# Pooled attention and two gated layers on one core: the first layer in blocks of 512 tokens instead of 288

## What is computed

```python
k_p = k.reshape(B, H, Sp, pool, D).mean(axis=3)
v_p = v.reshape(B, H, Sp, pool, D).mean(axis=3)
scores = scale * np.matmul(q, k_p.transpose(0, 1, 3, 2))
...
x = attn_out.transpose(0, 2, 1, 3).reshape(B * S, H * D)     # 4608 tokens x 512
h = x @ w_in                                                 # 512 -> 2048
g = np.where(h >= 1, h, np.where(h <= -1, 0.0, (h + 1) ** 2 / 4))
x = g @ w_out                                                # 2048 -> 512
h = x @ w_in2; g = h - np.tanh(h); y = g @ w_out2
```

## Time and profile before

| | us |
|---|---|
| median of 3 runs (1745.31 to 1745.89) | 1745.83 |
| the profiled execution | 1748.94 |
| its span, first to last instruction | 1747.0 |
| PE busy in it | 1709.3 (98%) |
| PE weight load busy | 1570.2 (90%) |
| DVE busy | 876.1 (50%) |
| ACT busy | 545.9 (31%) |
| POOL busy | 167.7 (10%) |
| mean granted TensorE clock | 0.993 of 2.4 GHz |
| chain that ended last, PE's share | 95% |

### The profile page before, as it was taken

The page is one execution under the profiler, slowest core; times in us unless marked ns, Lnnn a source line. Parts: engine busy times, 40 slices in busy tenths (PEclk is TensorE's granted clock), DMA queues, the critical chain, the costliest instruction groups (busy, mean ns, idle before and its releaser), DMA issues.

```text
span 1747.0 us, 24514 instructions
## 1 busy us (share of the span) xinstructions
PE 1709.3 (98%) x10480; PEld 1570.2 (90%) x10480; DVE 876.1 (50%) x1745; ACT 545.9 (31%) x1141; POOL 167.7 (10%) x136
## 2 busy tenths in 40 slices
PE   4999999999999999999999999999999999999998
PEld 4999999999999999999999888888888888888887
DVE  6585776767757768677554232323232323232322
ACT  3533333333333333333335222222222222222221
POOL 4610110011100110111007100000000000000000
PEclk7999999999999999999999999999999999999999
DMA  4512012002111020201024101010100000000000
GB/s 162 162 51 79 24 31 77 29 25 69 40 65 40 14 80 27 79 20 36 15 86 141 43 10 39 13 36 15 34 17 32 19 30 21 28 23 27 24 1 24
DMA packets 47628, 78.12 MB, mean 45 GB/s; under 512 B 3488, under 2 KB 19872, under 8 KB 47520
## 3 DMA queue, kind: packets, MB, share of 16 engines
q1 hardware_dynamic: 47520, 76.56, 13.5%
HBM read 57.67 MB, written 18.87 MB: 44 GB/s over the span
## 4 chain that ended last, share of the span: by engine, by line
PE 95%; DVE 3%; ACT 1%; POOL 0%; DMA 0%; issue 0%; DVEq 0%; SPq 0%
PE acc_ps L499 44%; PE h_ps L490 32%; PE att_ps L490 7%; PE score_ps L490 6%; PE score_ps L514 3%; PE score_ps L534 1%; PE att_ps L526 1%; DVE k_diag L850 1%; PE att_ps L534 0%; PE score_ps L535 0%; DVE g_lo L812 0%; DVE bent L819 0%; ACT bent L675 0%; DVE v_sum L861 0%; POOL win_lo L446 0%; DMA stage<-kT 0%
## 5 line engine op out<-in xcount | busy, mean ns | idle before, releaser
L499 PE MATMUL acc_ps<-g_hi,wout_hi 128*128 128x288 f32 (+1 forms) x1600 | 536.1, 335 | 2.1 <-DVE g_lo L812 2.1
L499 PE MATMUL acc_ps<-g_hi,wout_lo 128*128 128x288 f32 (+1 forms) x1600 | 526.0, 329 | 0.0
L499 PE MATMUL acc_ps<-g_lo,wout_hi 128*128 128x288 f32 (+1 forms) x1600 | 525.9, 329 | 0.0
L490 PE MATMUL h_ps<-x_hi,win_hi 128*128 128x288 f32 (+1 forms) x1248 | 400.9, 321 | 7.8 <-POOL win_lo L446 3.6
L490 PE MATMUL h_ps<-x_hi,win_lo 128*128 128x288 f32 (+1 forms) x1248 | 395.2, 317 | 0.0
L490 PE MATMUL h_ps<-x_lo,win_hi 128*128 128x288 f32 (+1 forms) x1248 | 395.1, 317 | 0.0
L499 PEld LDWEIGHTS acc_ps<-g_hi,wout_hi 128*128 128x128 f32 x1600 | 301.1, 188 | 25.4 <-DVE g_lo L812 2.4
L499 PEld LDWEIGHTS acc_ps<-g_lo,wout_hi 128*128 128x128 f32 x1600 | 301.1, 188 | 22.5
L499 PEld LDWEIGHTS acc_ps<-g_hi,wout_lo 128*128 128x128 f32 x1600 | 300.7, 188 | 22.3
L490 PEld LDWEIGHTS h_ps<-x_hi,win_hi 128*128 128x128 f32 x1248 | 234.9, 188 | 21.2 <-DVE g_lo L812 4.6
L490 PEld LDWEIGHTS h_ps<-x_lo,win_hi 128*128 128x128 f32 x1248 | 235.1, 188 | 11.2
(11 more groups left out here) (125 smaller groups left out, 1828.1 us busy)
## 6 DMA issues: line engine op xcount, KB each, us to landing
stage<-kT SPq DMA_DIRECT2D x16, 576.0 KB, 5.1
q_sb<-qT SPq DMA_DIRECT2D x16, 576.0 KB, 3.9
x2T_scratch<-prob SPq DMA_DIRECT2D x16, 576.0 KB, 3.4
x_lo<-x2T_scratch SPq DMA_DIRECT2D x9, 1024.0 KB, 7.3
yT<-out_sb SPq DMA_DIRECT2D x9, 1024.0 KB, 5.1
stage<-v SPq DMA_DIRECT2D x8, 1024.0 KB, 8.3
stage<-w_in SPq DMA_DIRECT2D x8, 1024.0 KB, 5.1
stage<-w_out SPq DMA_DIRECT2D x8, 1024.0 KB, 5.4
```

What stands on the lines that cost most here:

```text
L490: last = nc.tensor.matmul(h_bank(j, layer)[:, 0:WIDTH[layer]], w[:, c, j * P:(j + 1) * P], x[:, c, 0:WIDTH[layer]], start=(c == 0 and i == ...
L499: last = nc.tensor.matmul(acc_ps[:, m, 0:WIDTH[layer]], w[:, j, m * P:(m + 1) * P], g[:, j % GRING, 0:WIDTH[layer]], start=(j == 0 and i = ...
```

## The change

**Layer 1 in 9 blocks of 512 tokens.** T is 512 in both layers. Batches have 576 tokens, so a block no longer lies in one batch: block n holds the last 64 n tokens' worth of batch n - 1 and the first 512 - 64 n of batch n. `chunks(n)` cuts it into chunks of up to 128 queries of one batch: 4 where the border falls on a multiple of 128, else 5 (two of them of 64 queries); that is 5 for n = 1, 3, 5, 7 and 4 for the rest, 40 in all. `regions(n)` gives the one or two column ranges of a mix. Pooled K and V have two buffers, of the two batches.

**Attention.** Score units of a block use two PSUM banks in turn (`score_bank`), two units to a step from step 2. Turns and mixes stand at steps 9 to 14, the last three mixes and the last turn at steps 13 and 14. DVE makes `pool_k` in steps 0 and 1. POOL makes all of V's sums, by halving, tail included (`halve_v`), and DVE's `sum_v` is gone.

**x held once.** `x_hi` and `x_lo` have one buffer. `round_x1` of the next block waits until the last first product of this block is done.

**Weights where they land.** A piece of weights is loaded over the place of its low copy (`win_raw` and `win_lo` are the same memory); ACT casts it into the high copy and POOL subtracts in place. At the start SP issues all 8 pieces right behind K, Q and V, without a wait. In the last block of layer 1 a piece is loaded as soon as the piece that it replaces was last used. `q_sb` shares memory with the turned probabilities, so the next queries are loaded when the mixes are done.

```diff
-T = SEQ // 2
-BLOCKS = BATCH * SEQ // T
 TOKENS = BATCH * SEQ
-T2 = 512
-TP = 320
-LINE = 64
-BLOCKS2 = TOKENS // T2
-NEED2 = -(-T2 // T)
-CH = 96
-CHUNKS = T // CH
...
+T = 512
+BLOCKS = TOKENS // T
+SHIFT = SEQ - T
...
+def chunks(n):
+    edge = SHIFT * n
+    out = []
+    for c in range(T // P):
+        lo, hi = c * P, (c + 1) * P
+        if hi <= edge:
+            out.append((lo, P, n - 1))
+        elif lo >= edge:
+            out.append((lo, P, n))
+        else:
+            out.append((lo, edge - lo, n - 1))
+            out.append((edge, hi - edge, n))
+    return out
+def regions(n):
+    edge = SHIFT * n
+    return [r for r in [(0, edge, n - 1), (edge, T - edge, n)] if r[1] > 0]
...
-        x_hi = at("x_hi", X_AT, [P, 2, KT, TP], F32R)
-        x_lo = at("x_lo", X_AT + 2 * KT * TP, [P, 2, KT, TP], F32R)
...
+        win_raw = nc.alloc_sbuf_tensor_at("win_raw", [P, KT, FF], F32, offset=nc.lookup_mloc(win_lo.name).addr)
+        wout_raw = nc.alloc_sbuf_tensor_at("wout_raw", [P, FT, D], F32, offset=nc.lookup_mloc(wout_lo.name).addr)
+        x_hi = at("x_hi", X_AT, [P, KT, T], F32R)
+        x_lo = at("x_lo", X_AT + KT * T, [P, KT, T], F32R)
...
+        q_sb = at("q_sb", PT_AT, [P, PAIRS, T])
+        probT_hi = at("probT_hi", PT_AT, [P, PRING, T], F32R)
+        probT_lo = at("probT_lo", PT_AT + PRING * T, [P, PRING, T], F32R)
...
+        UNIT0_BANKS = [score_ps, h_ps[:, 0], h_ps[:, 1], acc_ps[:, 0], acc_ps[:, 1], acc_ps[:, 2], acc_ps[:, 3], att_ps]
+        def score_bank(n, k):
+            return UNIT0_BANKS[k] if n == 0 else [att_ps, score_ps][k % 2]
+        FIRST_STEPS = {0: 3, 1: 4, 2: 5, 3: 6, 4: 7}
+        SWITCH_STEPS = {2: 0, 5: 1, 6: 2, 9: 3, 10: 4, 13: 5, 14: 6}
...
             load_k(0)
-            load_q(0, 0)
+            load_q(0)
             load_v(0)
+            for i in range(NW):
+                load_w(1, i)
...
+            load_k(1)
+            sp.wait_ge(mixed, PAIRS)
+            load_q(1)
+            for blk in range(BLOCKS - 1):
+                n = blk + 1
+                if n < BATCH:
+                    sp.wait_ge(k_pooled, n + 1)
+                    load_v(n)
+                if n + 1 < BATCH:
+                    sp.wait_ge(v_split, n + 1)
+                    load_k(n + 1)
+                if n + 1 < BLOCKS:
+                    sp.wait_ge(mixed, PAIRS * (n + 1))
+                    load_q(n + 1)
                 store_out(blk)
...
+            def halve_v(b):
+                pool.wait_ge(v_loaded, 16 * (b + 1))
+                pool.wait_ge(v_tail_loaded, 16 * 2 * VTAIL_LOADS * (b + 1))
+                raw = v_raw(b).rearrange("p (i e) -> p i e", i=VTILES)
+                for level, width in enumerate([VE // 2, VE // 4, VE // 8]):
+                    if level > 0:
+                        pool.wait_ge(v_halved, 2 * b + level)
+                    if width > DH:
+                        nc.gpsimd.tensor_tensor(raw[:, :, 0:width], raw[:, :, 0:width], raw[:, :, width:2 * width],
+                                                ALU.add).then_inc(v_halved, 1)
+                    else:
+                        nc.gpsimd.tensor_tensor(v_sum[:], raw[:, :, 0:width], raw[:, :, width:2 * width],
...
-            for c in range(CHUNKS):
+            halve_v(0)
+            for c in range(len(chunks(0))):
                 normalise(0, c)
-            for i in range(4):
+            for i in range(6):
                 split_w(1, i)
-            normalise(1, 0)
-            split_w(1, 4)
-            normalise(1, 1)
-            split_w(1, 5)
-            normalise(1, 2)
-            split_w(1, 6)
-            split_w(1, 7)
-            for n in range(2, BLOCKS):
-                for c in range(CHUNKS):
+            for n in range(1, BLOCKS):
+                if n < BATCH:
+                    halve_v(n)
+                for c in range(len(chunks(n))):
                     normalise(n, c)
+                if n == 1:
+                    split_w(1, 6)
+                    split_w(1, 7)
...
+                    pe.wait_ge(k_pooled, min(n, BATCH - 1) + 1)
+                if n > 0 and k >= 2:
+                    pe.wait_ge(shift_done, GROUPS * before(n) + k - 1)
...
+                    last = nc.tensor.matmul(score_bank(n, k)[0:rows, e * 2 * KEYS:(e + 1) * 2 * KEYS],
+                                            q_sb[:, p, first:first + rows], k_diag[:, b % 2, p, :], start=True, stop=True)
...
+                for c, (first, rows, b) in enumerate(chunks(n)):
...
+                    last = nc.tensor.transpose(bank[:, first:first + rows], cols, ident[0:rows, 0:rows])
...
+                for first, cols, b in regions(n):
+                    at_ = slice(first, first + cols)
+                    for i, (w, x) in enumerate([(v_hi, probT_hi), (v_hi, probT_lo), (v_lo, probT_hi)]):
+                        nc.tensor.matmul(bank[:, at_], w[:, b % 2, p, :], x[:, p % PRING, at_], start=(i == 0), stop=False)
+                    last = nc.tensor.matmul(bank[:, at_], v_tail[:, b % 2, p, :], tailT[:, p // 2, at_], start=False,
+                                            stop=True)
+                last.then_inc(mixed, 1)
...
+            def attention(n, s, late):
+                units = GROUPS * len(chunks(n))
+                k = 2 * (s - 2) + int(late)
+                if 0 <= k < units:
+                    scores(n, k)
+                if s == 9 and not late:
+                    pe.wait_ge(tail_done, before(n + 1))
                     turn(n, TAIL_TURN, att_ps)
-                if point == 17:
-                    pe.wait_ge(norm_done, CHUNKS * (n + 1))
+                if s == 9 and late:
+                    pe.wait_ge(norm_done, before(n + 1))
                     turn(n, 1, score_ps)
-                if point == 18:
+                if s == 10 and not late:
                     pe.wait_ge(turn_split, TURNS * n + 1)
                     turn(n, 2, att_ps)
-                if point == 19:
-                    if v_b is not None:
-                        pe.wait_ge(v_split, v_b + 1)
+                if s == 11 and late:
+                    if n < BATCH:
+                        pe.wait_ge(v_split, n + 1)
                     mix(n, 0, score_ps)
-                if point == 20:
+                if s == 12 and not late:
                     pe.wait_ge(turn_split, TURNS * n + 3)
                     turn(n, 3, att_ps)
-                if point == 22:
+                if s == 13 and not late:
+                    pe.wait_ge(x1_split, PAIRS * n + 1)
+                    mix(n, 1, score_ps)
+                    pe.wait_ge(turn_split, TURNS * n + 4)
                     turn(n, 4, att_ps)
-                if point in (21, 23):
-                    p = 1 + (point - 21) // 2
-                    pe.wait_ge(x1_split, PAIRS * n + p)
-                    mix(n, p, score_ps)
-                if point == 24:
-                    pe.wait_ge(turn_split, TURNS * (n + 1))
+                if s == 14 and not late:
+                    pe.wait_ge(x1_split, PAIRS * n + 2)
+                    mix(n, 2, score_ps)
+                    pe.wait_ge(turn_split, TURNS * n + 5)
                     mix(n, 3, att_ps)
...
+            def round_x1(n, p, bank):
+                if n > 0 and p == 0:
+                    act.wait_ge(h_done, FT * n)
                 act.wait_ge(mixed, PAIRS * n + p + 1)
...
+            def block_body(blk, layer, att=None):
                 t0 = FT * blk
+                nch = len(chunks(att)) if att is not None else 0
                 for s in range(FT):
+                    ahead = 1 if blk + 1 < BLOCKS else 2
+                    if s + 1 < FT or blk + 1 < 2 * BLOCKS:
+                        split_gate(t0 + s + 1, (s + 1) % FT, layer if s + 1 < FT else ahead)
+                    if 0 <= s - 4 < nch:
+                        add_eps(att, s - 4)
+                    if att is not None and s == 10:
+                        split_turn(att, 1, score_ps)
+                    if s == 14:
+                        if att is not None:
+                            split_x1(att, 1, score_ps)
+                            split_turn(att, 4, att_ps)
+                            split_x1(att, 2, score_ps)
+                            split_x1(att, 3, att_ps)
+                        copy_sums(blk)
+                    if s + 2 < FT or blk + 1 < 2 * BLOCKS:
+                        now = layer if s + 2 < FT else ahead
+                        if now == 1:
+                            clip(t0 + s + 2, (s + 2) % FT)
+                        if 0 <= s - 4 < nch:
+                            invert(att, s - 4)
+                        if att is not None and s == 13:
+                            split_x1(att, 0, score_ps)
+                        if 0 <= s - 3 < nch:
+                            find_max(att, s - 3, 1)
+                            shift(att, s - 3, 1)
+                        gate(t0 + s + 2, (s + 2) % FT, now)
+                    if 0 <= s - 2 < nch:
```

(21 more changed lines are left out.)

718 lines of the change are left out of this document (274 added, 444 removed).

## The result

| | us |
|---|---|
| median of 4 runs (1727.58 to 1728.9) | 1727.84 |
| before beside it, median of 4 runs (1745.31 to 1748.85) | 1745.86 |
| ratio, 95% interval | 0.989 (0.988 to 0.991) |
| the profiled execution, its span | 1728.9, 1727.2 |

The change makes the kernel 1.1% faster. The forecast was 1702.5 with a range of 1694 to 1720: the sign is right, but the time is 25 us over the forecast and outside the range. Less than half of the expected gain came.

What follows compares the result with a forecast made beforehand. PE bounds it: matmul count times distance between starts. Span 1747.0 + 4.8 - 24.5 - 14.8 - 8.8 = 1703.7; execution 1.9 above, median 3.1 below that: 1702.5 us, own range 1695 to 1710, whole range 1694 to 1720.

Steps and rivals of the forecast that it cites:

- Layer 1's products, -24.5: Layer 1's product matmuls: 6144 at 0.1315 us become 3456 at layer 2's 0.2267, 808.0 us to 783.5.
- most of the fixed part stays: Rival, chance 0.01: wide layer-1 matmuls start 0.2318 us apart, 17.8 of the 24.5 us gone, time 1720.
- Attention beside the products, -14.8: Score units, turns and mixes between layer 1's product matmuls on PE: 99.6 us before, 84.8 after.
- The start, +4.8: Before the first product: first turn stays near 26 us, first product moves from 36.71 to 41.5; bounds +2 and +9.
- Block 0 and the switch, -8.8: Waits and cold clock from first product to layer 2: 13.8 us before, 5.0 stay (1.5 clock, 3.5 unplaced); bounds 1 and 14.
- The small waits for which 5 us were kept: Block 0 and the switch to layer 2: 1.5 us for cold clock and 3.5 us that couldn't be placed.
- 5 us to spare, cost nothing: V's halving moved to POOL: the fifth chunk's normalisation ends at 51.3 us, the first turn is at 56.4.
- POOL comes late: Rival, chance 0.07: V's halving and weights delay POOL, 5 us in block 0 and 1 us in odd blocks; time 1711.
- x held once: Block ends in layer 1: one buffer for x adds nothing; three spares of 1.1, 1.7 and 1.2 us.
- The third spare: Block end: x's last part is ready at 10.4 us, wanted by PE at 11.6, 1.2 to spare.
- the block's end leaks: Rival, chance 0.20: handovers or another DVE operation exceed the spare, 1 to 2 us in each of 8 blocks; 1710 to 1718.
- the slower one: Rival, chance 0.04: x splits can't hide under second products, 7.5 us at a block's end, 60 in 8 blocks; time 1762.

Runs made afterwards that it cites:

- e2: The changed kernel with score units always 128 queries wide, at batch borders too, DVE reading only its own rows: 1722.48 us.
- e3: The changed kernel with both 64-query border pieces in one 128-row slot, so every turn is four transposes of 128: 1722.65 us.
- e7: The changed kernel with the edits of e1, e2 and e3 together (1710.60 us), plus mixes uncut, the second batch's V left out: 1704.15 us.
- e8: The changed kernel with the edits of e1, e2 and e3 together (1710.60 us), plus POOL halving the first V in two parts: 1709.48 us.
- e1: The changed kernel with POOL's last two splits of layer 1's weights moved between chunks 1 to 3 of block 1's normalisation: 1721.53 us.
- e5: e1 plus two useless POOL additions with two SBUF inputs, behind the last normalisation of blocks 3, 5 and 7: 1733.61 us.

## Why the prediction was right or wrong

**Layer 1's products, -24.5: right.** 9 blocks at 87.05 are 783.4 (forecast 783.5), at the 0.2267 of layer 2. The rival by which most of the fixed part stays is out. The Trainium skill ("TensorE: Matmul & The Clock Gate", section "Back-to-back issue gap") gives a warm matmul its columns at 2.4 GHz and 2.5 ns, by an estimate 0.216 us at 512 columns; the rows show 0.2267, and more than the rule's at 288 columns too, so the measurement decides.

**Attention beside the products, -14.8: wrong, and the step that failed.** It was 105.5, not 84.8, and thus 5.9 dearer than the 99.6 of before. By its three terms:

| | forecast | measured | why |
|---|---|---|---|
| score units | 72 x 0.49 = 35.3 | 56 x 0.54 + 16 x 0.90 = 44.6 | "the same 144 columns, only more rows of queries, so 0.49 each" |
| turns | 40 x 0.46 = 18.4 | 20 x 0.47 + 20 x 0.79 = 25.2 | a transpose "0.07 to 0.10" at any width |
| mixes | 31.1 | 32 x 0.91 + 6.1 = 35.2 | a cut is paid by 4 x 9 ns, and by 0.5 more where a piece has 64 columns |
| sum | 84.8 | 105.0 | |

The sentence on score units looked only upward, from 96 queries to 128, and priced 16 units of 64 that the change makes for the first time by the same figure. The trace of before had no stationary side narrower than 96 beside the products, so this was an unknown cost; it was given one value and no bound. Whole turns were sized to 0.01, those with 64-row pieces not by themselves; by the distances above some 0.11 of their 0.32 more is the fifth transpose, and no run took the two apart. In the mixes the cut was seen and its size was off by 4: whole mixes at 0.91 are what the sum took, the cuts cost 6.1 and not 2. e2, e3 and e7 took these apart one by one: 0.36 a narrow unit (5.8 us for 16), 0.32 a turn (6.4 for 20) and 6.1 us. What they don't explain is the 0.05 by which a whole unit between 512-column products is dearer than one between 288-column ones (3.6 us in all). It lies in the matmuls from the third behind the unit on, as read above, and why they start late stays open.

**The start, +4.8: right to 1.** The first turn at 28.1 for 26, the first product at 42.4 for 41.5. POOL's chain began at 15.95, when V had landed, not at 13.5; but by e8 an earlier V wins little, since DVE's inverses are due next.

**Block 0 and the switch, -8.8: nearly right in size (7.0 stays, not 5.0), which is luck, and wrong in what stays.** The small waits for which 5 us were kept are not there: e1, without the stall, keeps about nothing. The 7.0 are one event that stood in the text as a cover: "5 us to spare, cost nothing" for V on POOL. The spare was counted for POOL's own queue, and there it held. It was not asked what POOL's two last splits, moved behind five chunks and V's halving, stand beside on DVE: V's placing, at the end of the same work. The rival "POOL comes late" named the place and, from "SBUF — State Buffer" of the Trainium skill, the rule, with 0.07 and a price for the wrong thing (late weights, 5 us), and its sentence that no row has two such operations side by side holds for the rows it read, not for the trace of before. There the start shows them, DVE's placing of the first V and POOL's normalisation:

```profile
23.41 1.92 DVE L872 TENSOR_TENSOR stage<-v_sum,own_tail 128x256 f32<-128x256 f32 x2
```

```profile
23.83 1.21 POOL L440 TENSOR_TENSOR prob<-prob,row_rcp 96x576 f32<-96x576 f32 x1
```

The second of the two small placings took 1.37 us and ended 0.3 after POOL's operation, where the median of that line is 0.41. It is the stall of the changed kernel in small.

**x held once: right.** PE had no wait for `x_lo` after the first block, in any of eight. The third spare can be read: `x_lo`'s last part ends 1.20 to 1.31 us before the first product behind it, where 1.2 was forecast. The likeliest rival (the block's end leaks, 0.20) gave 1710 to 1718 and did not happen, nor did the slower one.

**What was named as a check did its work**: 3456 matmuls 0.227 apart (yes), blocks of 98.5 and 97 (102 to 103, and 97.4 to 98.4), layer 2 at 915 (938.3), PE idle in layer 1 under 8 us (4.3). The first and the second together say at once that it is mostly attention in the five-chunk blocks that went wrong.

**The range** was made of the start's and the waits' bounds and of the leaking end. The term that held 20.7 us of error had none.

## What to carry to other kernels

When a change cuts work into pieces of a new shape, price the smallest piece by itself and give it a bound, for a narrower one can cost more than a whole one: padding 64 queries to 128, with half of the result unread, saved 0.36 us a unit, and filling a transpose's 128 rows from two pieces saved 0.32 a turn. When work moves from one engine to another, ask not only whether the new engine has time, but which operations with two SBUF inputs now run at the same moment on DVE and POOL; a DVE operation of 0.41 us took 4.7 on the mean beside POOL operations of 5. Together these repairs took the change from 1727.8 to 1710.6 us.

## What the hardware showed that was not expected

- Between 128-wide ones, a stationary operand of 64 columns was not loaded under the matmul ahead, with an idle PEld for 0.35 us, and neither was the 128-wide one behind it (0.20 us); one of 80, 96, 112 or 128 was. The Trainium skill ("TensorE: Matmul & The Clock Gate", section "Step-by-step: what each phase is for") has weight loads pulled ahead of running matmuls, on conditions of row groups or of a background buffer and none of width. The trace agrees from 80 columns on and inside a narrow unit, and disagrees at the change to 64 and back. Why is open.
- A POOL addition or subtraction of two SBUF inputs held a DVE multiplication of two SBUF inputs to its end (7.56 and 9.47 us for two that take 0.74). A POOL multiplication with one SBUF input, 5.4 to 5.8 us long, held one that ended 4.2 to 4.4 us after it began, and the next one then ran beside it in its usual 0.41.
- A wait of PE of 4.35 us cost 7.0, since the matmuls behind ran at 1.2 GHz (granted clock 0.83 over the stretch from 100 to 120 us). Of the shorter ones of e5, two did the same (2.33 us, matmuls 0.43 apart from 315.36 on, and 2.62); the third, again 2.33, did not (0.23 apart).
